# A fused attention and two-MLP kernel: output copies split around a step's first PSUM copies, step 2 and the last step reordered, the opening's loads in one row

## What is computed

```python
# q, k, v: (8 batches, 8 heads, 576 positions, 64)
k_p = k.reshape(B, H, 72, 8, D).mean(axis=3)
v_p = v.reshape(B, H, 72, 8, D).mean(axis=3)
scores = np.matmul(q, k_p.transpose(0, 1, 3, 2)) / sqrt(64)
attn = np.exp(scores - scores.max(axis=-1, keepdims=True))
attn = attn / (attn.sum(axis=-1, keepdims=True) + 1e-9)
x = np.matmul(attn, v_p)                      # as (4608 tokens, 512)
h = np.maximum(np.maximum(x @ w1, x @ w2), x @ w3)   # 768 wide
x = h @ w_out                                 # 512 wide
h = x @ w_in                                  # 2048 wide
g = h - np.tanh(h)
out = g @ w_out2                              # (4608, 512)
```

## Time and profile before

| | us |
|---|---|
| median of 3 runs | 1447.95 |
| lowest and highest run | 1446.58, 1449.45 |
| the profiled execution's own time | 1444.21 |
| its span in the trace | 1442.2 |
| PE busy in the span | 1425.7 |
| DVE, ACT, POOL busy | 1018.4, 661.4, 96.4 |

### The profile page before, as it was taken

The page is one execution under the profiler, slowest core; times in us unless marked ns, Lnnn a source line. Parts: engine busy times, 40 slices in busy tenths (PEclk is TensorE's granted clock), DMA queues, the critical chain, the costliest instruction groups (busy, mean ns, idle before and its releaser), DMA issues.

```text
span 1442.2 us, 26342 instructions
## 1 busy us (share of the span) xinstructions
PE 1425.7 (99%) x10794; PEld 1237.6 (86%) x10794; DVE 1018.4 (71%) x1765; ACT 661.4 (46%) x1291; POOL 96.4 (7%) x140
## 2 busy tenths in 40 slices
PE   8999999999999999999999999999999999999998
PEld 8888888888888878788898989989898988989897
DVE  7786666666666655534887777777777777777777
ACT  3322222222222221224666666566666666666655
POOL 2402121212121100000000000000000000000000
PEclk9999999999999999999999999999999999999999
DMA  6544444443534211145976665666666566575641
GB/s 225 199 165 135 174 137 171 136 172 121 188 120 156 85 74 38 74 175 214 353 262 229 236 238 212 233 227 224 250 216 250 207 226 248 203 267 205 210 175 52
DMA packets 81335, 269.74 MB, mean 187 GB/s; under 512 B 7168, under 2 KB 21504, under 8 KB 69568
## 3 DMA queue, kind: packets, MB, share of 16 engines
q1 hardware_dynamic: 81216, 268.07, 51.8%
HBM read 210.89 MB, written 57.15 MB: 186 GB/s over the span
## 4 chain that ended last, share of the span: by engine, by line
PE 92%; DVE 3%; DMA 2%; ACT 1%; issue 1%; SPq 0%; ACTq 0%; DVEq 0%
PE psum L678 29%; PE psum L718 26%; PE psum L740 23%; PE psum L692 10%; PE psum L621 2%; PE psum L661 2%; ACT out_stage L925 1%; DMA v_first<-in_v 0%; DMA w_mid_raw<-in_w_mid 0%; DMA w_raw<-in_w 0%; DVE poly L1144 0%; DVE poly L1160 0%; DVE probs L1072 0%; DVE h L1156 0%; DVE poly L1154 0%
## 5 line engine op out<-in xcount | busy, mean ns | idle before, releaser
L678 PE MATMUL psum<-x,w 128*128 128x512 f32 (+1 forms) x2160 | 452.7, 369 | 3.9 <-ACT first_copy L854 1.5
L678 PEld LDWEIGHTS psum<-x,w 128*128 128x128 f32 x2160 | 375.7, 188 | 75.2 <-ACT first_copy L854 1.7
L718 PE MATMUL psum<-w_out_s,g 128*128 128x512 f32 x1668 | 391.9, 390 | 0.4 <-DVE g L1139 0.4
L718 PEld LDWEIGHTS psum<-w_out_s,g 128*128 128x128 f32 x1668 | 308.6, 188 | 62.2 <-DVE g L1139 1.1
L740 PEld LDWEIGHTS psum<-x_even,ring 128*128 128x128 f32 x1680 | 208.4, 192 | 6.4 <-ACT copies L909 3.0
L740 PE MATMUL psum<-x_even,ring 128*128 128x256 f32 x1680 | 211.3, 283 | 2.2 <-ACT copies L909 2.2
L909 ACT ACTIVATE copies<-psum 128x256 f32<-128x256 f32 x288 | 108.2, 382 | 226.3 <-PE psum L740 224.9
L740 PE MATMUL psum<-x_odd,ring 128*128 128x256 f32 x1344 | 169.2, 283 | 2.2 <-ACT copies L909 2.2
L740 PEld LDWEIGHTS psum<-x_odd,ring 128*128 128x128 f32 x1344 | 166.5, 192 | 5.5 <-ACT copies L909 3.0
L862 ACT ACTIVATE h<-best 128x512 fp32r<-128x512 f32 (+1 forms) x60 | 35.3, 589 | 276.3 <-DVE best L1098 276.3
L692 PE MATMUL psum<-h,w_mid_s 128*128 128x512 f32 x648 | 151.7, 391 | 0.0
(11 more groups left out here) (82 smaller groups left out, 1027.8 us busy)
## 6 DMA issues: line engine op xcount, KB each, us to landing
ring<-w_scratch SPq DMA_DIRECT2D x72, 1024.0 KB, 7.2
ring<-w_scratch SPq DMA_DIRECT2D x72, 768.0 KB, 4.4
x_scratch<-x_stage SPq DMA_DIRECT2D x18, 1024.0 KB, 4.3
x_odd<-x_scratch SPq DMA_DIRECT2D x28, 512.0 KB, 5.7
x_even<-x_scratch SPq DMA_DIRECT2D x28, 512.0 KB, 5.5
x_scratch<-x_stage SPq DMA_DIRECT2D x18, 768.0 KB, 3.4
w_scratch<-w_stage SPq DMA_DIRECT2D x32, 384.0 KB, 2.6
v_raw<-in_v SPq DMA_DIRECT2D x21, 512.0 KB, 4.6
```

Of the source, the lines that this page charges most:

```text
L678: mm = pe.matmul(psum[:, bank, 0:hi - lo], w123[:, m, ws, n, c, :], x[:, xs, c, lo:hi], start=(c == 0 and ws + xs == 0), stop=(c == KC1 - ...
L718: mm = pe.matmul(psum[:, j, :], g_of(c)[:, gs, j * P:(j + 1) * P], w_out_s[:, row_of(c), ws, :], start=(m == 0 and gs + ws == 0), stop=(m ...
```

## The change

- **Output copies.** The four `drain_out` copies no longer stand together at the end of the step with p = 1: banks 0 and 1 stay there, banks 2 and 3 come in the next step, right behind `copy_sum(s, 3)`.
- **Step 2.** On DVE both `x2_sums` stand together, ahead of the GELU chunk. On ACT `x2_high` of the last chunk stands ahead of `g_hi(c, 0)`, where it stood behind it and behind `copy_sum(s, 2)`.
- **Last step.** `sum_third` stands ahead of `both_parts`. In the tail `mask` is behind `g_lo(c - 1, 1)`, and `g_lo(c, 0)` is ahead of the last `small_part`.
- **Opening, DVE and POOL.** The scaling of the first 128 tokens' probabilities is moved from DVE to POOL (`first_inv`, `first_normalized`); DVE sums the second 128 tokens meanwhile, and transposes them first. Three of nine warm-up matmuls go.
- **Opening, loads.** The wait of SP is gone, and pieces 4 to 7, the second batch's first keys and values and the first block of w_in are issued in one row; the keys come ahead of piece 3. `high` 6 and 7 move up in ORDER, from behind chunks 5 and (second half) 1 to behind chunks 3 and 5.

The diff, with unchanged lines cut:

```diff
@@ make_order
-        ("warm", 14), ("score", 0), ("score", 1), ("exp", 0), ("exp", 1), ("warm", 14), ("pool_v",), ("warm", 9), ("norm", 0), ("turn", 0),
-        ("high", 0), ("norm", 1), ("turn", 1), ("low", 0), ("attend", 0), ("high", 1), ("low", 1), ("high", 2)]
+        ("warm", 14), ("score", 0), ("score", 1), ("exp", 0), ("exp", 1), ("warm", 14), ("pool_v",), ("warm", 6), ("norm", 0),
+        ("high", 0), ("norm", 1), ("turn", 1), ("turn", 0), ("low", 0), ("attend", 0), ("high", 1), ("low", 1), ("high", 2)]
...
-                [("high", 5), ("turn", 3)], [], [("attend", 1)], [("high", 6)]]
+                [("high", 5), ("turn", 3)], [("high", 6)], [("attend", 1)], [("high", 7)]]
...
-            after_l1[1].append(("high", 7))
...
@@ SP
             load_q(3)
-            load_piece(3)
-
-            wait_filled(sp, ("l1", 0, 1, 0, HALF), NW - 1)
             for p in range(2):
                 load_k(1, p)
+            load_piece(3)
             load_piece(4)
-            load_piece(5)
             for p in range(2):
                 load_v(1, p)
+            for i in range(5, MC1 + 2):
+                load_piece(i)
+            load_w_raw(0)
 
             for entry in ORDER:
-                if entry == ("l1", 0, 4, 0, HALF):
-                    for i in range(MC1, MC1 + 2):
-                        load_piece(i)
-                    load_w_raw(0)
...
@@ POOL
+            pool.wait_ge(softmax_step, 3)
+            nc.gpsimd.tensor_tensor(probs[:, 0, :, 0:KEYS], probs[:, 0, :, 0:KEYS],
+                                    first_inv.unsqueeze(2).to_broadcast([P, GROUPS * 2, KEYS]), ALU.mult)\
+                .then_inc(first_normalized, 1)
...
@@ ACT step
                 copy_sum(s, 3)
+                if t > 0 and p == 2:
+                    drain_out(t - 1, (2, 3))
                 if s > 1:
                     g_hi(c - 1, 1)
...
                     shifted_square(c + 1, 1, 1)
+                if s == 2:
+                    x2_high(("l2", NT - 1, C_ORDER[3]))
+                if s > 0:
                     g_hi(c, 0)
                 act.wait_ge(multiplied, 6 * s + 6)
                 copy_sum(s, 2)
                 if t > 0 and p == 1:
-                    drain_out(t - 1, range(SUB))
-                if s == 2:
-                    x2_high(("l2", NT - 1, C_ORDER[3]))
+                    drain_out(t - 1, (0, 1))
...
@@ DVE
             def turn(n):
                 part = probs[:, n % 2, :, 0:KEYS]
-                dve.wait_ge(softmax_step, 4 * n + 3)
-                nc.vector.tensor_tensor(part, part, row_inv[:].unsqueeze(2).to_broadcast([P, GROUPS * 2, KEYS]),
-                                        ALU.mult).then_inc(softmax_step, 1)
-                dve.wait_ge(softmax_step, 4 * n + 4)
+                if n == 0:
+                    dve.wait_ge(first_normalized, 1)
+                else:
+                    dve.wait_ge(softmax_step, steps_before(n) + 3)
+                    nc.vector.tensor_tensor(part, part, row_inv[:].unsqueeze(2).to_broadcast([P, GROUPS * 2, KEYS]),
+                                            ALU.mult).then_inc(softmax_step, 1)
+                    dve.wait_ge(softmax_step, steps_before(n) + 4)
...
@@ DVE step
                 if s == 2:
                     x2_sums(("l2", NT - 1, C_ORDER[2]))
+                    x2_sums(("l2", NT - 1, C_ORDER[3]))
...
                 sum_second(s)
-                if s == 2:
-                    x2_sums(("l2", NT - 1, C_ORDER[3]))
+                if s == ALL2 - 1:
+                    sum_third(s)
                 if s > 0:
                     both_parts(c + 1, s - 1, 1, 1)
-                sum_third(s)
+                if s < ALL2 - 1:
+                    sum_third(s)
...
@@ DVE tail
-            mask(s, 1)
             small_part(c, 1, 0)
             g_lo(c - 1, 1)
+            mask(s, 1)
             both_parts(c, s, 1, 0)
...
             mask(s, 0)
+            g_lo(c, 0)
             small_part(c + 1, 0, 1)
-            g_lo(c, 0)
```

More of the change, by code:

```diff
@@ L300, in as_f32 @@
             return ap.bitcast(F32)
+        first_inv = row_max[:, 0]
         probs_zero = sem("probs_zero")
```

12 lines of the change are left out of this document (8 added, 4 removed).

## The result

| | before | changed |
|---|---|---|
| time, median of 5 runs (us) | 1447.95 (1446.58 to 1449.45) | 1433.57 (1433.14 to 1434.44) |
| profiled execution (us) | 1444.21 | 1433.14 |
| its span (us) | 1442.2 | 1431.3 |

The ratio of the times is 0.9903, 95% interval 0.9889 to 0.9916. The changed kernel is 14.4 us faster by the medians and 11.1 us by the two profiled executions. The prediction said 1439.7 us, in a range of 1437.0 to 1444.0: the direction was right, the size too small by 6.1 us.

The account below looks back on a forecast made before the run. PE was taken as the bound, busy 1425.7 of 1442.2 us, with 16.5 us idle. Terms 4.4 + 1.1 + 0.2 + 0.45 + 2.1 = 8.25 us off the median 1447.95 gave 1439.7 us, range 1437.0 to 1444.0.

Parts of the forecast that it names:

- What each edit can bring is capped by the wait it removes: All edited places: an edit gains at most the PE idle time shown there, such as 8 x 0.55 us for the output copies.
- the copies' term: Eight tiles' output copies: with two copies ahead, PE's wait of 0.55 us goes at each, 4.4 us (bounds 0 to 4.4).
- step 2: Second MLP, step 2: the bank is free before PE comes, so its wait goes, 1.1 us (bounds 0.6 to 1.1).
- The median of the runs stands 3.74 us above that execution: Sum: the 8.25 us gain is taken from the median 1447.95 us instead of the profiled 1444.21 us, giving 1439.7.
- The term for loads and pieces: Opening: PE's waits for ACT's copy, POOL's low part and DVE go, 1.5 + 0.4 + 0.2 = 2.1 us (bounds 0 to 2.3).
- Opening up to layer 1: Softmax work before layer 1: its first matmul starts 0.45 us earlier (bounds +0.45, and -1.0 if POOL takes twice the time).
- Rival (b): Opening: POOL's scaling takes twice 1.5 us, layer 1 starts 1.05 us later than before; 1441.2 us, chance 0.05.
- Loads and pieces, the part on what would be late: Opening, around 46 to 59 us: new POOL and DVE collisions, up to 1.2 us each, are costed at nothing.
- Rival (a): Opening, 30 to 60 us: POOL and ACT meet DVE's chain at new places and PE waits there; 1442.3 us, chance 0.16.
- Last step: End of the kernel: early `sum_third` removes 0.2 us of PE's 0.4 us wait if the last g does not move (bounds 0 to 0.45).
- (c): Output copies: the wait shrinks but stays, as the second PSUM copy or last product holds PE; 1441.9 us, chance 0.07.
- (d): Opening: early loads share bandwidth with pieces 1 to 3, up to 12.3 us later; slower, 1452.5 us at full size, chance 0.04.

## Why the prediction was wrong, step by step

**"What each edit can bring is capped by the wait it removes" failed, and with it the copies' term.** Each of the rows that were varied hides about 0.25 us more. The term of 8 x 0.55 = 4.4 us measured 8 x 0.80 = 6.4. The mechanism was right: the second PSUM copy ends in time, nothing is late behind `copy_sum(s, 3)`. The same constant makes step 2 1.33 us in place of 1.1. Together 2.3 us of the miss.

**"The median of the runs stands 3.74 us above that execution" was added as if it were fixed.** It wasn't. The profiled execution of before (1444.21 us) was one with a short wait for piece 4; most runs had a dip of the clock, and the four profiles with a long wait for piece 4 all have one. (The runs themselves have no trace; that theirs is the same dip is concluded.) The changed kernel has no such wait, and its runs lie within 1.3 us. The term for loads and pieces was read from that one execution at 2.1 us and got an upper bound of 2.3, the very waits shown; it measures 2.5 from that execution, 3.9 (2.2 to 5.5) added alone and 5.8 to 6.0 taken out. A little over half of the miss of 6.1 us, 3.3 us, is here: 14.4 won by the medians, 11.1 by the profiled executions. The constant above is 2.3, and what follows comes to 0.4 in sum.

**Opening up to layer 1.** 0.45 us forecast; 0.84 between the two profiles, of which 0.56 are the edit's and the rest is where PE stood ahead of it. This term and its parts were near. POOL scaled in 1.15 us (1.5 forecast), and the small DVE instruction beside it took 0.61 (0.9 forecast). Timeline of POOL and DVE in the changed kernel:

```profile
12.50 1.15 POOL L582 TENSOR_TENSOR probs<-probs,row_max 128x576 f32<-128x576 f32 x1 [10.38 <-DVE row_max L1079]
13.07 0.61 DVE L1076 TENSOR_SCALAR row_eps<-row_sum 128x8 f32<-128x8 f32 x1
```

It ends at 13.68, POOL at 13.65, while the row sum from 12.33 to 13.03 ran through at its 0.70 us. That agrees with the Trainium skill ("SBUF — State Buffer", section "Who interferes with whom"): a reduction is never held, and a tensor_scalar in a two-port mode waits for the whole GpSimd instruction. Rival (b) did not come.

**Loads and pieces, the part on what would be late.** I costed the new collisions at nothing and said PE would have no wait over 0.3 us between 20 and 75. It has one that ends at 30.37, of 1.25 us, which the trace gives to nobody. Rival (a) had PE wait in this stretch too, but for DVE and for twice as long. The wait appears in the second chunk of layer 1 in all six profiles with the loads in one row (0.97 to 1.83 us) and goes when that row is cut in two. So the cost that the sum lacked was not a collision of POOL and DVE: with the row of loads a 16 KB packet of the instruction queue starts 2.6 us later, and PE's wait ends 1.5 us after it. Still the forecast was too small and not too large, as the executions that it was measured against were worse than the one that I read.

**Last step.** 0.2 us forecast, -0.2 measured. That the last g might not move was seen; it moved back, behind the small parts, and the early `sum_third` (0.65 us) was spent on it. The g ends at 1423.93 + 0.63 = 1424.56 and PE starts 0.05 us later, so of the 0.2 us that the sum took for room some 0.15 were there before; but against the block of `between` ACT starts the last g 8.47 us after its start where it was 8.29.

**The rivals.** (c) did not come: with two copies ahead there was room, with three there would not have been. (d), the slower side, did not come either. Pieces 1 and 2, issued at 8.56 and about 9.0 us, landed after 9.3 and 10.7 us, at 17.9 and 19.7, where before they landed at 17.8 and 19.6. Piece 3 landed at 24.6 where it was 22.2, behind the keys that were put ahead of it, and ACT, which came to it at 24.86, didn't wait. The loads from the keys on took 11.8 to 19.9 us from issue to landing. The loads queued and did not share, which agrees with the Trainium skill ("DMA: Bandwidth & Descriptors", section "Queues, rings and completion order"): on each DMA engine descriptors are consumed in ring order. The experiment with piece 4 ahead of the keys shows the same from its bad side: 576 KB in front of a piece cost 3.0 us (1.7 to 4.2).

## What to carry over

Price a wait that recurs by the distance from block to block with it and without it, not by the idle time shown: here TensorE's waits of 0.55, 1.07 and 1.18 us were each worth 0.25 us more than their rows, and one of 0.32 us had no row at all. Where executions scatter, measure an edit from the last point that the scatter passes through, as the softmax edit here: 0.56 us in sixteen traces, where the runs showed nothing. Before a profiled execution is taken for the kernel, see where it lies among the runs; if it is one of the fast ones, look for a transfer whose landing decides a wait, since removing it is worth the median's wait and not the profile's. And when an order is changed at the end of a chain, look at the last instruction that the tail needs: it gains nothing if what was moved ahead of it takes what was won.

## What I had not expected of the hardware

- An issue of 768 KB behind 576 KB, onto idle queues, landed 4.6 to 7.4 us later in the six profiles that issue them so. The kernel before and the one with step 2 alone have the same program up to there, and they have 4.7 and 7.4. Why it spreads was not found.
- A full data queue seems to hold up TensorE's own instructions: with the loads in one row a 16 KB packet of the instruction queue started 2.6 us later and PE stood still for 0.97 to 1.83 us. That the packets carry PE's instructions is read from the queue's name and from the steady 1.28 to 1.60 us between a packet's end and PE's start. The same kind of wait stood at 66.26 us (1.17, DMA share 1.02 from 60 to 63 us) in the kernel with copies alone and at 59.60 us (1.20, share 1.03 from 54 to 56 us) in the one with piece 4 ahead, each 1.4 us after the end of such a packet. A full queue alone is not enough: with two groups of loads the share is 1.03 from 37 to 40 us and PE has no such wait, as no packet was due (they start at 29.8 and 45.5).
- A wait of 3.1 to 4.2 us in the opening was followed by 4 to 8 us at a granted clock of 0.50 to 0.85; one of 1.4 or 1.5 us by none. In the kernel with the softmax edit undone shorter ones did it too: behind 0.8 and 0.5 us of idle time the granted clock was 0.59 and 0.56 from 16 to 20 us, and around the wait of 1.83 us it was 0.79 from 30 to 36 us and 0.93 from 36 to 42. In the kernel with three copies ahead the two of 0.8 and 0.5 us did not.
